# Coarse attention as one run over 32 heads, with more buffers for raw rows and for the first tile's windows

## The reference

```python
q_d, k_d, v_d = mean over 4 neighbouring positions      # 144 rows a head
out_d = softmax(q_d @ k_d.T / 8) @ v_d                  # coarse, per batch and head
out_up = repeat(out_d, 4)
out_local = softmax(where(|i - j| < 4, q @ k.T / 8, -1e9)) @ v
x = (out_up + out_local) as [2304, 512]
xn = x / sqrt(mean(x*x) + 1e-6) * rms_g
x = (silu(xn @ w_gate) * (xn @ w_val)) @ w_out          # 512 -> 1536 -> 512
h = relu(x @ w_in); out = (s * h * h + b) @ w_out2      # 512 -> 2048 -> 512
```

## Time and profile before

| | |
|---|---|
| three runs | 1054.89, 1055.18, 1059.59 us, median 1055.18 |
| the profiled execution | 1056.84 us, its span 1054.7 us |
| PE busy | 958.6 us (91%) |
| DVE, POOL, ACT busy | 550.0, 406.8, 332.1 us |
| moved by transfers | 77.64 MB, 74 GB/s over the span |

### The profile page before, as it was taken

One profiled execution on the slowest core, in us unless ns is written; L12 is line 12 of the kernel. 1 busy time (PEld: TensorE's weight loads), 2 busy tenths in 40 slices (PEclk: granted clock), 3 DMA queues, 4 the chain that ended last, 5 costly groups with the idle time before them and its releaser, 6 DMA issues.

```text
span 1054.7 us, 13209 instructions
## 1 busy us (share of the span) xinstructions
PE 958.6 (91%) x5056; PEld 783.4 (74%) x5080; DVE 550.0 (52%) x807; ACT 332.1 (31%) x722; POOL 406.8 (39%) x203
## 2 busy tenths in 40 slices
PE   3764767799799999999999999999999999999997
PEld 2654656789677767777777889787888888888896
DVE  4577697777577567556554222334343443343343
ACT  2333355432422243233324144423222232222222
POOL 5855856778498658647460055300000000000000
PEclk9966658899899999999999999999999999999999
DMA  8555547524052123301100333201100200010010
GB/s 231 153 164 153 152 122 192 164 65 121 20 149 61 60 65 101 90 10 39 58 25 2 130 129 120 80 1 41 40 1 1 80 0 1 21 41 1 1 41 21
DMA packets 52046, 77.64 MB, mean 74 GB/s; under 512 B 6224, under 2 KB 33328, under 8 KB 51088
## 3 DMA queue, kind: packets, MB, share of 16 engines
q1 hardware_dynamic: 49968, 72.09, 23.0%
q10 hardware_dynamic: 2016, 4.72, 1.2%
HBM read 66.17 MB, written 10.62 MB: 73 GB/s over the span
## 4 chain that ended last, share of the span: by engine, by line
PE 75%; DVE 9%; POOL 6%; issue 3%; DMA 3%; ACT 2%; SPq 0%; DVEq 0%; ACTq 0%; POOLq 0%
PE bank L636 23%; PE bank L744 6%; PE bank L762 6%; PE bank L746 6%; PE bank L745 6%; PE bank L763 6%; PE bank L764 6%; PE bank L659 4%; PE bank L657 4%; PE bank L658 4%; POOL prod L460 3%; DVE sc L466 1%; POOL prod L446 1%; PE bank L1306 1%; DMA rawk<-in_k_dram 1%
## 5 line engine op out<-in xcount | busy, mean ns | idle before, releaser
L446 POOL TENSOR_TENSOR prod<-qs,ks 128x896 f32<-128x896 f32 x80 | 180.1, 2270 | 105.9 <-DVE sc L466 97.6
L460 POOL TENSOR_TENSOR prod<-sc,vs 128x896 f32<-128x896 f32 x80 | 153.2, 2015 | 71.9 <-DVE x L476 46.4
L783 DVE SCALAR_TENSOR_TENSOR r<-bank,r 128x512 f32<-128x512 f32 (+1 forms) x80 | 51.0, 638 | 183.9 <-ACT r L771 183.9
L746 PE MATMUL bank<-y_h,w2i_l 128*128 128x512 f32 (+1 forms) x320 | 117.9, 368 | 0.0
L657 PE MATMUL bank<-h_h,wo_h 128*128 128x256 f32 (+1 forms) x288 | 107.5, 373 | 0.0
L678 DVE TENSOR_TENSOR bank<-bank,u 128x256 f32<-128x256 f32 (+1 forms) x72 | 40.4, 561 | 124.6 <-PE bank L636 117.0
L636 PE MATMUL bank<-x_h,wv_h 128*128 128x256 f32 (+1 forms) x288 | 103.8, 376 | 0.0
L636 PE MATMUL bank<-x_h,wg_h 128*128 128x256 f32 (+1 forms) x288 | 93.9, 350 | 10.6 <-ACT u L666 6.4
L771 ACT ACTIVATE r<-bank 128x512 f32<-128x512 f32 (+1 forms) x80 | 44.4, 555 | 183.9 <-PE bank L746 183.2
L659 PE MATMUL bank<-h_h,wo_l 128*128 128x256 f32 (+1 forms) x288 | 98.0, 340 | 0.0
L658 PE MATMUL bank<-h_l,wo_h 128*128 128x256 f32 (+1 forms) x288 | 97.3, 338 | 0.0
(11 more groups left out here) (122 smaller groups left out, 1955.5 us busy)
## 6 DMA issues: line engine op xcount, KB each, us to landing
raww<-in_moe_w_out_dram SPq DMA_DIRECT2D x14, 512.0 KB, 3.9
rawk<-in_k_dram SPq DMA_DIRECT2D x4, 1152.0 KB, 6.1
rawq<-in_q_dram SPq DMA_DIRECT2D x4, 1152.0 KB, 6.5
rawv<-in_v_dram SPq DMA_DIRECT2D x4, 1152.0 KB
ks<-in_k_dram SPq DMA_DIRECT2D x16, 280.0 KB
vs<-in_v_dram SPq DMA_DIRECT2D x16, 280.0 KB
raww<-in_moe_w_in_dram SPq DMA_DIRECT2D x8, 512.0 KB, 3.6
y_raw<-y_scr SPq DMA_DIRECT2D x4, 1024.0 KB, 4.8
```

What stands on the lines that cost most here:

```text
L446: pool.tensor_tensor(dst, qv, kv, ALU.mult).then_inc(prod_ready, 1)
L460: pool.tensor_tensor(dst, pv, vv, ALU.mult).then_inc(prod_ready, 1)
L746: last = pe.matmul(o, w2i_l[:, m, kk, :], y_h[t % 2][:, kk, 0:w], start=False, stop=kk == DT - 1)
```

## The change

- **One run over heads.** The loops over batches and heads become one loop over `HEADS` = 32 heads. The transposed exponentials follow the scores two heads later (`TURN_LAG`), the product with v three heads later (`VAL_LAG`), also across batches. Scores have three banks of PSUM instead of two, `cs` has four places. The six units of the next batch's sums stand one a head, at heads 3 to 8 of the running batch, in one bank (`CTR`).
- **Raw rows in twelve places.** Each of four batches has its own place of raw q, k and v (of v, batch 3 shares that of batch 0). They lie where weights lie later, so the first weights wait for all sums (`q_pooled`, `k_pooled`, `v_pooled`).
- **Sums of v through DRAM.** Raw v is loaded over all 128 partitions instead of 72, summed to `vd` in two instructions, stored to `v_scr`, and loaded back as `dv`, 72 partitions by 16 runs of 64 values.
- **Four places for tile 0's windows** (`qs2`, `ks2`, `vs2`); the second pair lies in `raww` and in weights, so the first piece of weights is loaded after tile 0's last product of q and k.
- **Other places of the work around it:** the norm of tile 0 takes one inverse root for all four slices; POOL makes the low part of pieces 0, 1, 2 and six more, after tile 0; tile 1's products begin behind them; in chunk 0 DVE's `split_lo` stands ahead of the weights; `finish_pooled` divides four heads at a time.

```diff
+HEADS = B * H
+TURN_LAG, VAL_LAG = 2, 3
+UNIT_FROM = 3
+QK0_AT = {0: (0,), 1: (1,), 2: (2,), 3: (3,), 4: (4,), 5: (5,), 6: (6,), 7: (7,), 8: (8, 9), 9: (10, 11), 11: (12,), 12: (13, 14), 13: (15,)}
+PV0_AT = {16: (0, 1), 17: (2, 3), 18: (4,), 19: (5, 6), 20: (7,), 21: (8, 9), 22: (10,), 23: (11, 12), 24: (13, 14), 25: (15,)}
...
-QK1_AT = {0: (2, 3), 1: (4,), 2: (5,), 3: (6, 7), 4: (8,), 5: (9, 10), 6: (11,), 7: (12,), 8: (13,), 9: (14, 15)}
+QK1_AT = {0: (0, 1), 1: (2, 3), 2: (4,), 3: (5, 6), 4: (7,), 5: (8,), 6: (9,), 7: (10, 11), 8: (12,), 9: (13, 14), 10: (15,)}
...
-        CTR, CSC, CPT, COB = bank[4:6], bank[0:2], bank[2:4], bank[6:8]
+        CTR, CSC, CPT, COB = bank[5], [bank[0], bank[1], bank[4]], bank[2:4], bank[6:8]
+        CTR0 = [bank[5], bank[2], bank[3]]
...
             def load_rawk(b):
-                wait(sp, k_pooled, b)
-                sp.dma_start(rawk[:, :, :], k_rows[b]).then_inc(rawk_loaded, 16)
+                sp.dma_start(rawk[b][:, :, :], k_rows[b]).then_inc(rawk_loaded[b], 16)
...
+            def store_vd(b):
+                sp.wait_ge(v_pooled, b + 1)
+                sp.dma_start(v_scr[b].rearrange("(p t) d -> p t d", p=P), vd[:, :, :]).then_inc(vd_stored, 16)
+
+            def load_dv(b):
+                sp.wait_ge(vd_stored, 16 * (b + 1))
+                wait(sp, cpv, H * (b - 1))
+                sp.dma_start(dv[0:JH, b % 2, :, :], v_scr[b].rearrange("(n p) d -> p n d", p=JH)).then_inc(dv_loaded[b % 2], 16)
...
             load_qk(sp, 0, 0)
+            load_rawv(0)
             load_qk(sp, 0, 1)
-            load_rawv(0)
+            load_rawk(1)
+            load_rawq(1)
             load_qk(sp, 0, 2)
...
+            store_vd(0)
+            load_rawv(1)
+            load_qk(sp, 0, 3)
+            load_dv(0)
...
             for n in range(16):
-                if n == KPOOL_AT[2] - 16:
-                    pool_k(3)
                 pv_mult(pool, 0, n)
-            for n in range(4):
-                qk_mult(pool, 1, n)
+            weight_lo(pool, 0)
+            weight_lo(pool, 1)
             weight_lo(pool, 2)
...
+            for n in range(HEADS + VAL_LAG):
+                if n < HEADS:
+                    b, h = divmod(n, H)
+                    third = ((h + 1) * J - 1) // (3 * P)
+                    wait(pe, cexp, 2 * (n - 2))
+                    pe.wait_ge(ctr_evac, UNITS * b + 2 * third + 2)
...
+                if TURN_LAG <= n < HEADS + TURN_LAG:
+                    g = n - TURN_LAG
+                    pe.wait_ge(cexp, 2 * (g + 1))
...
+                if n >= VAL_LAG:
+                    g = n - VAL_LAG
+                    b, h = divmod(g, H)
+                    pe.wait_ge(cpt_evac, g + 1)
+                    if h == 0:
+                        pe.wait_ge(dv_loaded[b % 2], 16 * (b // 2 + 1))
+                        wait(pe, co_ready, 2 * b - 1)
...
+                b, i = divmod(n - UNIT_FROM, H)
+                if 0 <= b < B - 1 and i < UNITS:
+                    turn_pooled(b + 1, i)
```

More of the change, by code:

```diff
@@ L347, in weight_hi @@
             act.wait_ge(raww_loaded[n % SLOTS], 16 * (n // SLOTS + 1))
+            if n < 2:
+                act.wait_ge(q_pooled, B)
+                act.wait_ge(k_pooled, B)
+                act.wait_ge(v_pooled, B)
+            if n == FIRST_ORDER.index(("out", 0)):
+                act.wait_ge(cpv, HEADS)
             if n >= NW1:
@@ L1056, in _ @@
                     split_bf(act, c + 1, 1)
-                if c == 0 and m == 10:
-                    softmax_exp(act, 1)
-                if c == 1 and m == 5:
-                    squares(act, 1, 0)
-                if c == 1 and m == 7:
-                    squares(act, 1, 1)
-                if c == 1 and m == 8:
-                    normalise(act, range(FAC), 3)
                 if 2 <= c < NCH - 1:
@@ L1072, in _ @@
                     if m == 9 + late:
-                        normalise(act, range(FAC), 2 + c)
+                        normalise(act, range(FAC), 1 + c)
                 if (c, m) in ROUND_AT and ROUNDS[c + 1] > 2:
@@ L1091, in _ @@
                     split_bf(act, 1, m - 4)
+                if c == 0 and m == 11:
+                    softmax_exp(act, 1)
+                if c == 1 and m == 4:
+                    squares(act, 1, 0)
+                if c == 1 and m == 6:
+                    squares(act, 1, 1)
+                if c == 1 and m == 7:
+                    normalise(act, range(FAC), 2)
                 if c == 1 and m in ROUNDS_1:
@@ L1164, in finish_pooled @@
+            def finish_pooled(b, g):
+                dve.wait_ge(cexp, 2 * (H * b + 4 * g + 4))
+                cb = csum[0:JH, b % 2, 8 * g:8 * g + 8]
+                c_link(dve.tensor_scalar(cb, cb, 1e-9, float(FAC), ALU.add, ALU.mult))
+                c_link(dve.reciprocal(cb, cb))
+                wait(dve, co_stored, 16 * b)
                 dve.wait_ge(cpv, H * b + 4 * g + 4)
@@ new lines, in _ @@
+            pool_q(0, 0)
+            pool_q(0, 1)
+            pool_v(0, 0)
+            pool_v(0, 1)
+            for n in range(HEADS):
+                b, h = divmod(n, H)
+                dve.wait_ge(csc_ps, n + 1)
+                wait(dve, cexp, 2 * (n - H + 1))
+                dve.tensor_reduce(cneg[0:JH, h, :], CSC[n % 3][0:JH, 0:2 * J].rearrange("p (a j) -> p a j", a=2),
+                                  op=ALU.min, axis=AX.X).then_inc(cneg_ready, 1)
+                for i in QK0_AT.get(n, ()):
+                    qk_reduce(dve, 0, i)
+                for i in PV0_AT.get(n, ()):
+                    pv_reduce(dve, 0, i)
+                if b < B - 1 and h < 2:
+                    pool_q(b + 1, h)
+                if b < B - 1 and 2 <= h < 4:
+                    pool_v(b + 1, h - 2)
+                if b and h == 4:
+                    finish_pooled(b - 1, 1)
+                if h == 7:
+                    finish_pooled(b, 0)
+                if n == 13:
@@ L1232, in _ @@
                 if c == 0:
+                    if m in (4, 5):
+                        split_lo(dve, 1, m - 4)
                     for n in LO_AT.get(m, ()):
```

420 lines of the change are left out of this document (207 added, 213 removed).

## The result

The changed kernel takes 1041.3 us (1040.24 to 1042.42 in 4 runs) beside 1055.74 us before: the ratio is 0.9856, with an interval of 0.9829 to 0.9884. It is faster, by 14.4 us instead of the 35.7 that I forecast, and 3.3 us above my range. The profiled run has a span of 1039.8 us.

What follows compares the result with a forecast made beforehand. It took the three stretches ahead of chunk 2 as where time could be won, PE being full after. Start 131, chunk 0 69, chunk 1 57.2 and the rest 761.8 gave 1019.0 us of span, so 1019.4; range 1003 to 1038.

Steps and rivals of the forecast that it cites:

- Let go at 33: Start: PE waits for batch 0's `dv`, back through DRAM, until 33 us (ends 29 and 40).
- PE's chain, 95.3 us of work: Start, after `dv`: scores, transposes, products and units take 93.8 us at 1.2 GHz; with the row turn, PE ends at 128.3.
- Two chains of one length wait for each other now and then; I add 2 us.: Start: PE's and POOL's chains both end near 129; with 2 us of mutual waits the first gate begins at 131.
- The step on POOL's chain: Start: POOL's sums, products and waits for tile 0 end at 110; the work behind them ends at 129 us.
- Chunk 0 at 69: First layer chunk: shorter waits ahead of step 2 and for `x_l`, net 7 us, give 69 instead of 76.0.
- The term for tile 1's late products: Chunk 0: only two of four tile 1 products done by the gate, pieces 8 to 11 asked for late; 2 us lost.
- Chunk 1 at 57.2: "later start and denser order cancel.": Chunk 1: tile 1's later softmax and denser sums per step cancel; left at 57.2 us, ends 51 and 63.
- The rest: From chunk 2's first gate to the end: order kept, 761.8 us unchanged.
- C: Rival, start: PE's queue stops at late minima as DVE waits for POOL's product; gate 140, total 1038 us; chance 0.22.
- B: Rival, start: PE granted 2.4 GHz, gate 127, 1015 us; 997 if chunk 0 also runs at PE's pace; chance 0.14.
- D: Rival, start: DRAM round trip of v's sums replaces each batch's end; batches stay 34 us, time 1055; chance 0.05.
- E: Rival, chunk 0: weight pieces pass one at a time, 8.9 us each, 124 us for 14; total 1074; chance 0.04.

Runs made afterwards that it cites:

- the last kernel: Changed kernel without the scaling, units evicted before exponentials, tile 1's work and windows rescheduled, POOL's first tile 1 product waiting for tile 0's inverse root: 1017.89 us, ratio 0.9627.

## Why the prediction was wrong

**Let go at 33.** Right: 32.65, and not by errors that cancel. The sums of v were done at 19.0 (estimate 19.5), `dv` was asked for at 25.6, when the store had landed (26), and it was there at 32.65.

**PE's chain, 95.3 us of work.** Right: from 32.65 to 142.49 are 109.84 us, less 12.8 of waits 97.0. Heads are 2.73 and 3.37 apart, at 1.2 GHz.

**"Two chains of one length wait for each other now and then; I add 2 us."** This step failed: 12.8 us. The added 2 counted only waits that two busy engines give each other by order, and DVE, "no third chain", had no term of its own. I took durations of DVE's instructions from a start in which POOL often stood, and did not ask which of them would grow once POOL worked on beside them. The step on POOL's chain failed by the same cause: its last product of tile 0 ended at 119.3 and not at 110 (I had named 118 as the mark). With the scaling out it ended at 111.9; POOL's waits for DVE's sums of products with v went from 7.4 us to 0.3. That 111.9 lies so close to 110 is luck in part: POOL still waited 12.0 us for the sums of q times k, where I allowed 4, but only 2.1 for the softmax, where I had 7.2, and its products were shorter (2.22 and 2.02 us, not 2.41 and 2.15). The stretch from tile 0's last sum to the gate was mis-sized too: 22.0 us (120.5 to 142.5) and not 18.9; with the inverse root free of POOL it is 18.7 (112.7 to 131.4). That last gate, at 131.4, is close to the forecast of 131, but by edits that the forecast did not have.

The rows speak first: five of eight scalings took 1.03 to 3.30 us while POOL was at work, and end within 0.04 us of an end of POOL's work (a product in four cases, the low part of a weight in one); the three that met POOL idle or between two products took 0.16. The reciprocal took 0.19 beside POOL. The Trainium skill, "SBUF — State Buffer", section "Who interferes with whom", has the rule behind it: a vector instruction with two inputs in SBUF, or one like `tensor_scalar` in a mode that uses both ports, and an instruction of GpSimd (POOL here) that reads SBUF exclude each other for a whole instruction, while one with at most one input in SBUF and outside these modes does not wait. By that rule a price of the change could have been seen from the order of its instructions: each `tensor_scalar` that moves beside POOL's products costs up to a product. Whether the scaling ran in such a mode no run here shows. The trace agrees with the exclusion, and adds that the wait can be longer than one instruction: at 78.58 it lasted through two products in a row.

**Chunk 0 at 69.** Measured 72.25. Both waits that I had removed shrank, that of 4.2 to 1.7 (by 2.5, where I had counted 3) and that of 6.4 to 0.6 (by 5.8, counted 4). The term for tile 1's late products, 2 us, was too small: POOL stood for 20.39 us, SP stood with it at a window until 156.8, piece 8 was asked for at 159.2, ACT waited for it until 163.35, and from that come the 3.9 us; the 3.8 end with POOL's low part of piece 13 (193.77 us).

**Chunk 1 at 57.2: "later start and denser order cancel."** This step failed: 63.19. POOL's first product with v of tile 1 stood 4.7 us ahead of chunk 1's first `hidden_mul` before (first two rows), and 0.2 behind it with the change (last two):

```profile
231.04 7.13 POOL L460 TENSOR_TENSOR prod<-sc,vs 128x896 f32<-128x896 f32 x4 [4.85 <-DVE sc L505]
```

```profile
235.70 0.42 DVE L678 TENSOR_TENSOR bank<-bank,u 128x256 f32<-128x256 f32 x1
```

```profile
214.90 10.83 POOL L522 TENSOR_TENSOR prod<-sc,vs 128x896 f32<-128x896 f32 x6 [2.64 <-DVE sc L567]
```

```profile
214.74 0.42 DVE L740 TENSOR_TENSOR bank<-bank,u 128x256 f32<-128x256 f32 x1
```

A denser order of DVE's sums gives nothing back, since POOL makes a product in about 2 us whatever the order. The run with half of POOL's work, and the two with whole products that start earlier, speak for this chain as what sets the beginning of chunk 2.

**The rest.** Right: 761.87.

**The rivals.** C (lockstep: gate at 140, chunk 0 as before, tile 1 late in chunk 1, 1038 us) was the nearest to what happened, with 142.5, 72.3 and 63.2. It had the place right, late minima in DVE's queue, and gave as cause a sum that waits for its product; it is DVE's small instructions that wait. It should have had more than 0.22, and its upper end should have stood above 1038. B fell: 0.50 from 33 us to the gate of the changed kernel, and the same with PE busy for 115 us without a gap. The Trainium skill, "TensorE: Matmul & The Clock Gate", section "HAM oscillation", explains a low clock by pauses; that run had none, so the measurement decides, and here the absence of pauses was not enough. D fell: after 32.65 PE waits for no `dv` in the changed kernel. But with two window places it came true for batch 2: how far SP's queue is held up decides it. E fell: chunk 0 took 72.25 us and not over 105. Piece 8 alone went through load, high and low part in a row, 8.4 us (159.21 to 167.63), close to the 8.9 that E had.

What stays open: how much of the gain from half of POOL's work is its length alone, which of the last moves of tile 1 brought how much, and what sets chunk 0's 72.95 us in the last kernel, of which PE is busy for 61.33.

## What to carry to other kernels

When a change lets two engines work at the same time that took turns before, take each short instruction's duration again: ask whether it may be held by the other engine, and what is queued behind it. A transfer queue that mixes kinds of loads is as slow as the place that its front entry waits for, so more places for one kind can pay off in another. A wait removed in one stage is a gain only if the next stage's inputs are not the later ones; find the chain that lets the next stage begin and shorten that.

## What the runs showed of the hardware that was not expected

- A DVE `TENSOR_SCALAR` of 72x8 takes 0.16 us alone and up to 3.30 beside POOL's products; `RECIPROCAL` of the same tile takes 0.18 to 0.20 in both cases, and `TENSOR_REDUCE` from SBUF takes its 1.07 us with POOL at work.
- POOL is held as well: a product of 1.80 us took 3.78 beside DVE's sum of two halves of raw q (128x1152).
- PE's clock stayed at 0.50 through 115.00 us of unbroken work with small products and four dense ones a head.
- The granted clock in a row can mislead: the last kernel's start shows 1.00, and PE is busy there for 105.12 us, as in the changed kernel at 0.58 (104.39); a head with a unit takes 3.37 us in both.
